# Attention by blocks of two heads, 64 queries and 96 columns, in an attention and two-layer mixture kernel

## What is computed

```python
# attention: q, k, v are (2, 8, 768, 64); 8 memory keys and values per head
scores = scale * np.matmul(q_c, k_full.transpose(0, 1, 3, 2))   # per chunk of 32 queries
scores = scores - np.max(scores, axis=-1, keepdims=True)
a = np.exp(scores)
a = a / (np.sum(a, axis=-1, keepdims=True) + 1e-09)
out[:, :, c_start:c_end] = np.matmul(a, v_full)
# dense: x (1536, 512), w_in (512, 2048), w_out (2048, 512)
h = x @ w_in
g = h * (1.0 / (1.0 + np.exp(-1.702 * h)))
x = g @ w_out
# experts: argmax of x @ w_gate, then relu(x @ w1[e]) @ w2[e], scaled by the gate
```

## Time and profile before

| | |
|---|---|
| median of 3 runs | 579.5 us (578.07 to 580.6) |
| profiled execution | 577.89 us, its span 576.2 us |
| PE busy | 550.5 us, 96% |
| DVE, ACT, POOL busy | 299.7, 246.0, 170.0 us |
| first product of the dense outputs (end of the attention) | 96.34 us from the span's start |

### The profile page before, as it was taken

One profiled execution on the slowest core, in us unless ns is written; L12 is line 12 of the kernel. 1 busy time (PEld: TensorE's weight loads), 2 busy tenths in 40 slices (PEclk: granted clock), 3 DMA queues, 4 the chain that ended last, 5 costly groups with the idle time before them and its releaser, 6 DMA issues.

```text
span 576.2 us, 8715 instructions
## 1 busy us (share of the span) xinstructions
PE 550.5 (96%) x3156; PEld 460.6 (80%) x3156; DVE 299.7 (52%) x580; ACT 246.0 (43%) x530; POOL 170.0 (30%) x207
## 2 busy tenths in 40 slices
PE   7999998999999999999999999988999999899993
PEld 6878866888888887888887788778989888798882
DVE  5887875444423334322355544614444467856850
ACT  3766774334323222221343434302655367674620
POOL 1534430000000000200000110020667469999942
PEclk9999999999999999999999999979999999999997
DMA  8788623990000000100123342335759185985100
GB/s 235 218 259 240 222 73 112 342 277 2 1 0 2 0 1 1 73 1 0 38 81 103 103 154 73 110 110 163 226 203 318 63 324 180 326 301 191 50 25 29
DMA packets 28138, 75.31 MB, mean 131 GB/s; under 512 B 5423, under 2 KB 5551, under 8 KB 28080
## 3 DMA queue, kind: packets, MB, share of 16 engines
q1 hardware_dynamic: 23808, 67.96, 35.9%
q0 software_dynamic: 3840, 6.32, 3.0%
q10 hardware_dynamic: 432, 0.28, 0.2%
HBM read 61.90 MB, written 18.91 MB: 140 GB/s over the span
## 4 chain that ended last, share of the span: by engine, by line
PE 87%; issue 3%; DVE 3%; POOL 3%; DMA 2%; ACT 1%; SPq 0%; POOLq 0%; DVEq 0%; ACTq 0%
PE bank L1083 10%; PE bank L1085 10%; PE bank L1084 10%; PE bank L1127 8%; PE bank L1129 8%; PE bank L1128 8%; PE bank L1040 4%; PE bank L1096 4%; PE bank L1074 3%; PE bank L1076 3%; PE bank L1298 3%; PE bank L1299 3%; PE bank L1300 3%; PE bank L1198 2%; PE bank L1051 2%
## 5 line engine op out<-in xcount | busy, mean ns | idle before, releaser
L319 POOL TENSOR_TENSOR w_lo<-raw,w_hi 128x256 fp32r<-128x256 f32 x100 | 85.9, 895 | 43.6 <-ACT w_hi L303 43.5
L466 POOL DMA_INDIRECT dispatched_rows<-rows,slot_idx x12 | 11.9, 992 | 286.6 <-DVE slot_idx L867 283.9
L766 DVE SCALAR_TENSOR_TENSOR g<-g,bank 128x512 f32<-128x512 f32 x48 | 33.0, 687 | 111.4 <-ACT g L544 111.4
L544 ACT ACTIVATE g<-bank 128x512 f32<-128x512 f32 x48 | 28.8, 599 | 135.8 <-PE bank L1085 135.8
L303 ACT ACTIVATE w_hi<-raw 128x1024 fp32r<-128x1024 f32 x80 | 82.8, 1052 | 0.1
L1127 PE MATMUL bank<-w_hi,g_hi 128*128 128x512 f32 x192 | 76.0, 396 | 1.5 <-issue 1.5
L1083 PE MATMUL bank<-x_hi,w_hi 128*128 128x512 f32 x192 | 76.8, 400 | 0.0
L319 DVE TENSOR_TENSOR w_lo<-raw,w_hi 128x1024 fp32r<-128x1024 f32 x55 | 72.2, 1312 | 8.7 <-ACT w_hi L303 8.6
L1129 PE MATMUL bank<-w_hi,g_lo 128*128 128x512 f32 x192 | 75.8, 395 | 0.0
L1128 PE MATMUL bank<-w_lo,g_hi 128*128 128x512 f32 x192 | 75.7, 394 | 0.0
L1085 PE MATMUL bank<-x_hi,w_lo 128*128 128x512 f32 x192 | 75.6, 394 | 0.0
(11 more groups left out here) (126 smaller groups left out, 1046.5 us busy)
## 6 DMA issues: line engine op xcount, KB each, us to landing
raw<-expert_units SPq DMA_DIRECT2D x64, 512.0 KB, 5.1
raw<-dense_units SPq DMA_DIRECT2D x16, 512.0 KB, 5.4
dispatched_rows<-empty SPq DMA_DIRECT2D x24, 257.0 KB, 12.1
slot_rows<-dispatched_rows SPq DMA_DIRECT2D x24, 257.0 KB, 4.2
tile_in<-attention_tiles SPq DMA_DIRECT2D x12, 512.0 KB, 3.6
tile_in<-attention_tiles SPq DMA_DIRECT2D x12, 320.0 KB, 5.6
tile_in<-attention_tiles SPq DMA_DIRECT2D x24, 128.0 KB, 4.8
out<-rows,e_token POOLq DMA_INDIRECT x24, 4.7
```

What stands on the lines that cost most here:

```text
L319: last = engine.tensor_tensor(w_lo[u % RING][:, part], raw[u % RING][:, part], w_hi[u % RING][:, part].bitcast(F32), ALU.subtract)
L766: dve.scalar_tensor_tensor(g32[i % 2][:, :], g32[i % 2][:, :], 1.0, h_bank[i % 2][:, :], ALU.add, ALU.mult).then_inc(s_g, 1)
```

## The change

A product becomes two heads by 64 queries, against 96 columns: 88 positions and 8 memory keys. The queries are laid out in runs of 128 columns, in which 64 queries of the even head and 64 of the odd one stand side by side, each with zeros in the other's partitions. A tile has again 8 blocks: 4 pairs of heads by 2 windows. The keys of a tile stand once, with the memory keys at both ends; the values are stored per window, 96 partitions by 512, twice.

- Scores: 8 products of 96 columns. Two sets of two PSUM banks take turns by tile, where before three banks served all tiles.
- DVE adds the mask in two pieces of 384 elements and takes the maximum of 768 (in two pieces for tile 0). It no longer scales the maximum, no longer copies transposed probabilities, and now sums the probabilities itself (768 elements, in `inverse`).
- GpSimd adds the negated maximum to the masked scores (`less_max`, two instructions a tile), and multiplies by the inverse in two instructions. It does `less_max(t + 1)` ahead of `normalise(t)`.
- ACT takes one exponential per four blocks (384 elements, no bias, no accumulated sum), and copies both halves of the transposed probabilities.
- PE transposes 8 blocks of 96 columns, and `values` is 16 products, each with 64 columns of weights and 64 moving columns, two per block into the two halves of the output partitions.
- Queries are now written in runs of 512 B (five or four of them a partition), where a partition's queries were one run of 2,048 B. Keys: 2,688 B a partition in place of 2,560. Values: 96 partitions of 4,096 B in place of 128.

```diff
-    HPB = 3
-    GROUPS = [(g, min(g + HPB, H)) for g in range(0, H, HPB)]
+    HALF = P // 2
+    WINDOWS = P // HALF
+    KEYS = HALF + LEFT + RIGHT + M
+    SPAN = P + LEFT + RIGHT + 2 * M
+    NBL = NP * WINDOWS
+    BPG = NBL // 2
+    GROUPS = [(g, g + BPG) for g in range(0, NBL, BPG)]
...
-        score_bank, pTa_bank, pTb_bank, xT_bank = bank[0:3], bank[3:5], bank[5], bank[6:8]
+        score_bank, pT_bank, xT_bank = (bank[0:2], [bank[2], bank[5]]), bank[3:5], bank[6:8]
...
+        def query_runs(n, half, odd):
+            runs = NP if odd else NP + 1
+            part = tile_in[n][half * D:(half + 1) * D, odd * P:odd * P + runs * 2 * P]
+            return part.rearrange("p (c x) -> p c x", x=2 * P)[:, :, 0:P]
...
-                    sp.dma_start(tile_in[n][at_, half * Q_IN:(half + 1) * Q_IN], attn_in[t, at_, 0:Q_IN])\
+                    there = attn_in[t, half * D:(half + 1) * D, 0:(NP + 1 - half) * P]
+                    sp.dma_start(query_runs(n, half, half), there.rearrange("p (c x) -> p c x", x=P))\
                       .then_inc(s_qk[n], 16)
...
-                sp.dma_start(tile_in[n][:, QK:ATT], attn_in[t, :, ATT - 2 * DM - Q_IN:ATT - Q_IN])\
-                  .then_inc(s_v[n], 16)
+                there = attn_in[t, 0:KEYS, Q_IN + NP * SPAN:Q_IN + NP * SPAN + WINDOWS * DM]
+                sp.dma_start(tile_in[n][0:KEYS, QK:ATT], there).then_inc(s_v[n], 16)
...
+            def less_max(t):
+                for g, (x0, x1) in enumerate(GROUPS):
+                    for n, some in enumerate(MAX_GROUPS[t]):
+                        if some[0] == x0:
+                            pool.wait_ge(s_max, max_done(t, n))
+                    part = masked[t % 2][:, x0:x1, :]
+                    pool.tensor_tensor(part, part, by_row(neg_max[t % 2], x0, x1), ALU.add).then_inc(s_sub, 1)
+
+            def normalise(t):
+                pool.wait_ge(s_inv, t + 1)
+                for x0, x1 in GROUPS:
+                    part = prob[t % 2][:, x0:x1, :]
+                    pool.tensor_tensor(part, part, by_row(prob_inv[t % 2], x0, x1), ALU.mult).then_inc(s_norm, 1)
...
-                    last = act.activation(prob[t % 2][:, h, :], masked[t % 2][:, h, :], ACT.Exp,
-                                          bias=exp_bias[t % 2][:, h:h + 1], scale=SCALE,
-                                          accum_out=prob_sum[t % 2][:, h:h + 1])
+                for g, (x0, x1) in enumerate(GROUPS):
+                    act.wait_ge(s_sub, NG * t + g + 1)
+                    act.activation(prob[t % 2][:, x0:x1, :], masked[t % 2][:, x0:x1, :], ACT.Exp, scale=SCALE)\
+                       .then_inc(s_exp, 1)
...
             def inverse(t):
-                dve.wait_ge(s_exp, t + 1)
+                dve.wait_ge(s_exp, NG * (t + 1))
...
+                dve.tensor_reduce(prob_sum[t % 2][:, :], prob[t % 2][:, :, :], AX.X, ALU.add).then_inc(s_sum, 1)
...
             def scores(t):
-                    if t:
-                        pe.wait_ge(s_mask, NG * (t - 1) + g + 1)
+                    if t >= 2:
+                        pe.wait_ge(s_mask, NG * (t - 2) + g + 1)
...
-                    pe.matmul(dst, vb[:, cols], probT_b[t % 2][:, 2 * c // 4, :], start=True, stop=False)
-                    for h in (2 * c, 2 * c + 1):
-                        last = pe.matmul(dst[h % 2 * D:(h % 2 + 1) * D, :], va[:, h * D:(h + 1) * D],
-                                         probT_a[t % 2][:, h, :], start=False, stop=True)
+                for x in range(NBL):
+                    c, w = divmod(x, WINDOWS)
+                    if x % BPG == 0:
+                        pe.wait_ge(s_pTa, NG * t + x // BPG + 1)
+                    for half in range(2):
+                        v0 = QK + w * DM + (2 * c + half) * D
+                        side = (half + w) % 2 * HALF
+                        last = pe.matmul(xT_bank[t % 2][half * D:(half + 1) * D, x * HALF:(x + 1) * HALF],
+                                         tile_in[n][0:KEYS, v0:v0 + D],
+                                         probT[t % 2][0:KEYS, x, side:side + HALF], start=True, stop=True)
```

More of the change, by code:

```diff
@@ L446, in _, with by_row @@
                                base=-1, pattern=[[1, P]], channel_multiplier=-1).then_inc(s_pool_c, 1)
-            for t in range(NT):
-                pool.wait_ge(s_inv, t + 1)
-                if t >= 2:
-                    pool.wait_ge(s_pT, 3 * (t - 1))
-                for g in range(2):
-                    part = prob[t % 2][:, 4 * g:4 * g + 4, :]
-                    inv = prob_inv[t % 2][:, 4 * g:4 * g + 4].rearrange("p (h a) -> p h a", a=1)
-                    rest = prob_b[t % 2][:, 4 * g * KB:4 * (g + 1) * KB].rearrange("p (h k) -> p h k", k=KB)
-                    pool.tensor_tensor(rest, part[:, :, P:KEYS], inv.to_broadcast([P, 4, KB]), ALU.mult)
-                    pool.tensor_tensor(part[:, :, 0:P], part[:, :, 0:P], inv.to_broadcast([P, 4, P]), ALU.mult)\
-                        .then_inc(s_norm, 1)
+            def by_row(stats, x0, x1):
+                return stats[:, x0:x1].rearrange("p (x a) -> p x a", a=1).to_broadcast([P, x1 - x0, KEYS])
+            def less_max(t):
[10 more added lines that the diff above has]
+                    pool.tensor_tensor(part, part, by_row(prob_inv[t % 2], x0, x1), ALU.mult).then_inc(s_norm, 1)
+            less_max(0)
+            for t in range(NT):
+                if t + 1 < NT:
+                    less_max(t + 1)
+                normalise(t)
             pool.wait_ge(s_fill, 16 * (SLOTS // P))
@@ L775, in _ @@
                 for half in range(2):
[L776 to L777 removed]
+                    dve.memset(query_runs(n, half, 1 - half), 0.0).then_inc(s_zero_q, 1)
             for t in range(-3, NT + 1):
[L779 removed]
+                if 0 <= t + 1 < NT - 1:
                     inverse(t + 1)
[L781 to L782 removed]
                 if t == NT - 1:
@@ L1412 @@
     T, NT, TPB, KT = B * S, B * S // P, S // P, DM // P
-    win = P + LEFT + RIGHT
-    keys = win + M
+    half = P // 2
+    keys, span = half + LEFT + RIGHT + M, P + LEFT + RIGHT + 2 * M
+    q_in = (H // 2 + 1) * P
     f32 = np.float32
-    def pairs(a):
-        return np.ascontiguousarray(a.transpose(0, 2, 1, 3)).reshape(a.shape[2], H // 2, 2 * D).transpose(2, 1, 0)
-    attn = np.zeros((NT, P, H // 2 * P + H // 2 * keys + 2 * DM), f32)
+    attn = np.zeros((NT, P, q_in + H // 2 * span + 2 * DM), f32)
@@ L1425 @@
     for t in range(NT):
         b, s0 = t // TPB, t % TPB * P
-        qt = pairs(q[b:b + 1, :, s0:s0 + P])
+        qt = q[b, :, s0:s0 + P].transpose(0, 2, 1)
+        attn[t, 0:D, half:half + H // 2 * P] = qt[0::2].transpose(1, 0, 2).reshape(D, -1)
+        attn[t, D:P, 0:H // 2 * P] = qt[1::2].transpose(1, 0, 2).reshape(D, -1)
         lo, hi = max(0, s0 - LEFT), min(S, s0 + P + RIGHT)
-        kw = np.zeros((1, H, keys, D), f32)
-        vw = np.zeros((H, keys, D), f32)
-        kw[0, :, lo - s0 + LEFT:hi - s0 + LEFT] = k[b, :, lo:hi]
@@ L1432 @@
-        kw[0, :, win:] = mem_k[b]
-        vw[:, lo - s0 + LEFT:hi - s0 + LEFT] = v[b, :, lo:hi]
-        vw[:, win:] = mem_v[b]
-        va = vw[:, 0:P].transpose(1, 0, 2).reshape(P, DM)
-        vb = np.zeros((4, keys - P, H, D), f32)
-        for h in range(H):
-            vb[h % 4, :, h] = vw[h, P:]
-        attn[t] = np.concatenate([qt.reshape(P, -1), pairs(kw).reshape(P, -1), va,
-                                  vb.reshape(P, DM)], axis=1)
-    mask = np.full((P, 3, keys), -1e30, f32)
@@ L1444 @@
-    for r in range(P):
-        u0 = r // CHUNK * CHUNK
-        mask[r, :, u0:u0 + LEFT + CHUNK + RIGHT] = 0.0
-    mask[:, 0, 0:LEFT] = -1e30
-    mask[:, 2, P + LEFT:win] = -1e30
-    mask[:, :, win:] = 0.0
+        kw = np.zeros((H, span, D), f32)
+        vw = np.zeros((H, span, D), f32)
+        for wide, own, memory in ((kw, k, mem_k), (vw, v, mem_v)):
+            wide[:, M + lo - s0 + LEFT:M + hi - s0 + LEFT] = own[b, :, lo:hi]
+            wide[:, 0:M] = memory[b]
+            wide[:, span - M:] = memory[b]
@@ new lines @@
+        attn[t, :, q_in:q_in + H // 2 * span] = kw.reshape(H // 2, 2, span, D).transpose(1, 3, 0, 2).reshape(P, -1)
+        for w in range(2):
+            at = q_in + H // 2 * span + w * DM
+            attn[t, 0:keys, at:at + DM] = vw[:, w * (half + M):w * (half + M) + keys].transpose(1, 0, 2).reshape(keys, DM)
+    mask = np.full((P, 3, 2, keys), -1e30, f32)
+    for r in range(P):
+        u0 = r % half // CHUNK * CHUNK
+        for w in range(2):
+            at = M * (1 - w) + u0
+            mask[r, :, w, at:at + LEFT + CHUNK + RIGHT] = 0.0
@@ L1453, in in_units @@
+    mask[:, 0, 0, M:M + LEFT] = -1e30
+    mask[:, 2, 1, keys - M - RIGHT:keys - M] = -1e30
+    mask[:, :, 0, 0:M] = 0.0
+    mask[:, :, 1, keys - M:] = 0.0
+    mask = mask.reshape(P, 3, 2 * keys)
     def in_units(w):
```

149 lines of the change are left out of this document (53 added, 96 removed).

## The result

The changed kernel takes 571.5 us (median of 4 runs, 570.0 to 572.7), the kernel before beside it 580.1 (4 runs, 578.1 to 582.4). The ratio is 0.985, with a 95% interval of 0.980 to 0.990: faster by 8.5 us, where 22.8 were forecast, and outside the range of 547 to 567. The profiled execution took 572.34 us, its span is 570.6. Ratios leave out executions more than 1.5% above the fastest of their kernel; medians and ranges are of all runs.

A forecast was written before the change was run, and what follows sets the result against it. PE was taken to bound the attention at 6.37 us a tile, the loads afterwards at 5.5. Tile 11's queries at 55.5 plus 18.0 us put dense outputs at 73.5, not 96.34: 22.8 off 579.5 gives 556.7 us, range 547 to 567.

The forecast's parts named there:

- PE's tile: PE in the attention loop: transposes 0.92, scores 1.8, values 1.1, together 3.8 us a tile in place of 6.37.
- Rival 2: Attention's value passes don't shrink: PE's tile stays at 5.6 us, total 569 us; chance 0.10.
- DVE, ACT, POOL: Smaller engines in the attention loop: 4.2, 2.9 and 3.3 us a tile, ACT and POOL hidden.
- rival 5: The change brings nothing: a chain through POOL waits every tile until a tile takes over 6 us; chance 0.02.
- DMA: Attention loads: 5.5 us for a tile with its weight unit, becoming the bound; tile 11's queries land at 55.5 us.
- Bytes against partitions: Values' load in the attention, priced by bytes: 0.393 MB a tile taking 1.28 us.
- rival 1: Attention loads keep up, queries costing 0.96 us a tile: dense outputs at 68.8, total near 551.5 us; chance 0.19.
- Packets of 512 B: Attention's query loads: 576 packets a tile at 38 ns each, 1.37 us; over 60 ns would refute the forecast.
- rival 3: Every query packet costs what a 2 KB packet costs: dense outputs at 104.6, total 587.8 us, slower; chance 0.03.
- The clock: PE's granted clock in the attention was to stay at 1.00.
- Rival 4: PE idles 1.7 of 5.5 us and its clock falls: attention ends at 110.7, total 594 us; chance 0.02.
- A microsecond won before 96.34 should be a microsecond of the total.: After the attention nothing is touched, so all 22.8 us gained before the first dense output reach the total.

The follow-up runs named there:

- e5: Changed kernel with values loaded into all 128 partitions, the extra rows being zeros, in place of 96: 567.3 us, ratio to the kernel before 0.976.
- e3: Changed kernel with queries loaded for tiles 0 to 2 only, later tiles reusing them, so results are wrong: 557.7 us.
- e12: Changed kernel with 20 idle products ahead of PE's wait for the queries of tiles 6 to 11: 574.0 us.
- e14: Changed kernel with 9 warm products at the start in place of 75, moving PE's later code back to its old place: 571.3 us.

## Why the prediction failed

*PE's tile.* Right: 3.85 us for 3.8, with scores at the price of 128 columns of weights (1.86) and values that shrank to 1.08. Rival 2 is out.

*DVE, ACT, POOL.* Right: 3.75, 2.38 and 3.23 us a tile for 4.2, 2.9 and 3.3. No wait for `prob` in the middle of the loop; rival 5 is out.

*DMA.* The right mechanism, and the step that failed is its rate. "307 GB/s when busy" was read from the loads of the kernel before and used to price loads of new shapes, which gave 5.5 us for a tile with its unit. For the old shapes it was sound: the stretch had 251 GB/s at a share of 0.84, 299 for each full share, and up to 346 where the share was near 1. The new shapes had 257 at 1.08, 238 for each full share, and 6.05 us for a tile with its unit (1.556 MB). With 14.7 MB ahead of tile 11's queries (12 x 0.639 + 9 x 0.393 + 6 x 0.524 + 0.33) in 52.8 us the forecast counted on 278 GB/s; the engines moved 249 up to 64.26 us, and some 0.8 of these 15.5 MB (184 packets of 4096 B beyond the 1632 due) were loads behind tile 11's queries, a term that the forecast didn't have. It had the queries at 55.5; PE got them at 64.26, 8.8 late. From there the forecast had 18.0 to the first output and it took 20.1, in part at half clock (64.9 to 71.8). The two make the 10.9 between 73.5 and 84.37. PE's waits were uneven, 0.46 to 2.38 us, where some 1.3 each was forecast.

*Bytes against partitions.* The change sent fewer bytes for values by loading 96 of 128 partitions, and I took 1.28 us by bytes for 1.71. That saving does not exist (e5), and the load to 96 partitions made the units beside it slower. With every load spread over 128 partitions and the units three tiles later the kernel takes 555.4. That this is near the forecast's 556.7 is luck, for it is another kernel; there the loads nearly keep up, which the forecast had as rival 1. (Rival 1's sum, 96.34 - 68.8 off 579.5, is 552.0 and not 551.5.)

*Packets of 512 B.* I took 38 ns, the records show 44; rival 3, and the sentence that 60 ns would refute me, looked at the packets' own time. What they cost their neighbours is a rival left open: without them the rate rose to 283 GB/s (e3).

*The clock.* Forecast 1.00, measured 0.86 in the loop after waits of 1.7 and 2.2 us. Rival 4's cause was there and cost at most some 1.1 us at the first output (e12).

*"A microsecond won before 96.34 should be a microsecond of the total."* Of 12.0 us 8.5 arrived. The code that moved has the first expert's code fetched later (e14 against all others); that this costs the 1.6 us is likely and not shown. The rest lies in an expert stage whose length differs by 3.6 us between two profiles of one kernel.

*The start.* First transposes at 18.97 and, repeated, 15.76, where 16.4 was forecast: it varies by 3.2 us, and the first outputs differ by 0.4.

## What to carry to other kernels

A rate read from one kernel's loads holds for loads of those shapes. Before you price new ones with it, look at which partitions they fill and how long their packets are. Here a load to 96 partitions saved nothing over 128 and slowed its neighbours; zeros that completed it, and one wide load in place of narrow ones in runs of 512 B, were together worth 13 us. A zero loaded raises the GB/s and is no work done, so judge by the time. Before you blame a fallen clock, fill the wait with idle products; and profile the kernel before twice, for a stage with branches differed by more than a third of the gain.

## What the runs showed that was not expected

- The DMA engines moved 257, 298, 294 and 420 GB/s in the same stretch at shares of 1.02 to 1.08: with narrow queries and 96-partition values, with full values, with wide queries, with both. Without the added zeros these are an estimated 257, 275, 247 and 330.
- 133 more instructions on PE, far from the experts, moved the fetch of the first expert's code from 8.7 and 11.0 to 3.6 to 4.1 us before its first product.
- One DVE instruction of 1.2 us lasted 7.33 beside twelve of GpSimd, and a cast of 0.15 us lasted 6.31.
